# The second feed-forward product as seven block products per pair of row and column halves, in place of eight

## The reference

```python
def _moe_ref(x, phi, w1, w2):            # x: 3072 tokens x 512
    logits = x @ phi                     # 32 slots
    ...                                  # 8 experts, 4 slots each
    c = exp(logits - max); c /= c.sum(1)
    return c @ slot_out

def _moe2_ref(x, w_in, w_out):           # w_in 512 x 2048, w_out 2048 x 512
    h = x @ w_in
    r = np.maximum(h, 0.0)
    g = r * r
    return g @ w_out
```

## Time and profile before

| what | value |
|---|---|
| median of 3 runs | 565.27 us (564.38 to 565.62) |
| the profiled execution, device time | 565.99 us |
| its span in the profile | 564.0 us |
| TensorE busy in the span | 520.0 us, 92% |
| VectorE / ScalarE / GpSimd busy | 291.5 / 274.9 / 107.1 us |
| first matmul of the second product | 273.13 us |
| last matmul of the kernel starts | 560.32 us |
| 256 tokens of the last stage, steady | 24.0 us |

### The profile page before, as it was taken

How to read it: one execution, slowest core, us unless ns; L and a number is a source line. 1 busy time by engine, 2 the same in 40 slices (tenths; PEclk the granted TensorE clock), 3 DMA queues, 4 the chain that set the end, 5 groups by cost and what they waited for, 6 DMA issues and landing times.

```text
span 564.0 us, 10786 instructions
## 1 busy us (share of the span) xinstructions
PE 520.0 (92%) x3477; PEld 400.6 (71%) x3477; DVE 291.5 (52%) x909; ACT 274.9 (49%) x722; POOL 107.1 (19%) x230
## 2 busy tenths in 40 slices
PE   2899999999999688676899999999999999999997
PEld 1677877888788522311788888888888888888886
DVE  4676676676776542302797444444443543544410
ACT  1677777777877310001766443443443444444420
POOL 1444444444444203300260000000000000000000
PEclk9999999999999979797999999999999999999999
DMA  6699945535644679998001000000000000000000
GB/s 256 231 403 405 405 161 186 193 126 153 206 144 129 224 294 397 387 387 321 1 0 40 20 22 33 19 19 19 19 37 19 19 19 19 19 37 19 19 20 37
DMA packets 25993, 77.01 MB, mean 137 GB/s; under 512 B 2416, under 2 KB 2416, under 8 KB 23408
## 3 DMA queue, kind: packets, MB, share of 16 engines
q1 hardware_dynamic: 21776, 64.10, 31.6%
q10 hardware_dynamic: 4192, 12.58, 5.9%
HBM read 70.39 MB, written 6.29 MB: 136 GB/s over the span
## 4 chain that ended last, share of the span: by engine, by line
PE 69%; DVE 8%; ACT 5%; issue 5%; POOL 4%; SPq 4%; DMA 3%; ACTq 0%; DVEq 0%; POOLq 0%
PE bank L1091 14%; PE bank L1090 14%; PE bank L1089 14%; PE bank L860 5%; PE bank L871 5%; POOL probs L385 4%; ACT probs L719 4%; PE bank L1076 4%; SPq L338 4%; PE bank L903 2%; DMA w_b<-w_dram 2%; PE bank L886 2%; PE bank L1038 1%; DVE g_s L688 1%; DVE probs L478 1%
## 5 line engine op out<-in xcount | busy, mean ns | idle before, releaser
L1091 PE MATMUL bank<-wo_hi,g_lo 128*128 128x512 f32 x352 | 138.6, 394 | 0.0
L1090 PE MATMUL bank<-wo_lo,g_hi 128*128 128x512 f32 x352 | 138.1, 392 | 0.0
L1089 PE MATMUL bank<-wo_hi,g_hi 128*128 128x512 f32 x352 | 137.4, 390 | 0.0
L688 DVE TENSOR_TENSOR g_s<-relu_s 128x512 f32<-128x512 f32 x96 | 69.4, 729 | 129.5 <-ACT relu_s L814 129.5
L814 ACT ACTIVATE relu_s<-bank 128x512 f32<-128x512 f32 x96 | 56.3, 596 | 124.3 <-PE bank L1076 124.2
L719 ACT ACTIVATE probs<-probs,nmax 128x232 f32<-128x232 f32 (+1 forms) x192 | 88.6, 463 | 50.5 <-DVE nmax L478 50.5
L385 POOL TENSOR_SCALAR probs<-probs,rden 128x232 f32<-128x232 f32 (+1 forms) x192 | 82.5, 448 | 104.3 <-DVE rden L487 104.3
L1091 PEld LDWEIGHTS bank<-wo_hi,g_lo 128*128 128x128 f32 x352 | 66.2, 188 | 14.1
L1090 PEld LDWEIGHTS bank<-wo_lo,g_hi 128*128 128x128 f32 x352 | 66.1, 188 | 11.9
L1089 PEld LDWEIGHTS bank<-wo_hi,g_hi 128*128 128x128 f32 x352 | 66.2, 188 | 11.6
L691 DVE TENSOR_TENSOR g_lo<-g_s,g_hi 128x512 fp32r<-128x512 f32 x96 | 68.7, 722 | 4.5
(11 more groups left out here) (129 smaller groups left out, 507.6 us busy)
## 6 DMA issues: line engine op xcount, KB each, us to landing
qkv_s<-qkv_dram SPq DMA_DIRECT2D x16, 1028.0 KB, 5.7
qkv_s<-qkv_dram SPq DMA_DIRECT2D x16, 704.0 KB, 4.1
w_s<-w_dram ACTq DMA_DIRECT2D x5, 2048.0 KB, 11.9
w_s<-w_dram SPq DMA_DIRECT2D x6, 1024.0 KB, 13.4
out_dram<-o_stage SPq DMA_DIRECT2D x24, 256.0 KB, 2.0
w_a<-w_dram SPq DMA_DIRECT2D x9, 512.0 KB, 10.9
wo_raw<-w_out_dram SPq DMA_DIRECT2D x4, 1024.0 KB, 14.3
w_pre<-w_dram ACTq DMA_DIRECT2D x1, 2048.0 KB, 18.0
```

The costliest lines, as they stand in the source:

```text
L688: dve.tensor_tensor(g_s[:, j % 4, :], relu_s[:, j % 4, :], relu_s[:, j % 4, :], ALU.mult).then_inc(squared, 1)
L1089: pe.matmul(bank[4 + q][:, :], hi, wo_hi[:, f, :], start=(f == 0), stop=False)
L1090: pe.matmul(bank[4 + q][:, :], hi, wo_lo[:, f, :], start=False, stop=False)
L1091: last = pe.matmul(bank[4 + q][:, :], lo, wo_hi[:, f, :], start=False, stop=(f == FFC - 1))
```

## The change

The matrix product of 256 tokens (two halves of 128, A1 and A2) x 2048 with w_out is written as 2 x 2 blocks: the token halves against the halves of the 16 blocks (u = 0, 1: a11, a12 for the first 128 tokens, a21, a22 for the second), and w_out against the halves of its rows and of its 512 columns. Seven block products of sums and differences replace the eight plain ones (Winograd's form of Strassen's scheme). The four combinations of w_out blocks (`t_32`, `t_hi`, `t_lo`) are made once. The four combinations of g blocks (`s_32`) are made for each pair of token tiles.

A block product has 256 output columns. The 16 blocks of hidden columns of a pair are worked in two groups (c = 0, 1) of 4 blocks of either half. A group is 7 products x 4 blocks x 3 matmuls = 84 matmuls of 256 columns, and 8 `hidden` matmuls of 256 columns for the pair after it, 4 behind its third product and 4 behind its fifth. So a pair of tiles has 168 + 16 matmuls of 256 columns, in place of 96 of 512 and 16 of 256. The first pair (`plain`) is computed with the plain eight products, since the w_out combinations are made beside it.

ScalarE's program becomes: the high parts of group G (`a_hi` for both plain blocks, then `s_hi` slots 0 to 4), then `gate` of group G + 2: ReLU of 1024 columns out of PSUM twice, then two squares in place of 1024 columns each, now on ScalarE too. VectorE makes three of the four combinations of g, `a_lo` and four of the five `s_lo` slots, and adds the seven products up to the output tiles (`outputs`, seven operations of 256 columns, PSUM against SBUF). GpSimd makes for every group the combination a11 - a21 and the low part of the slot 4. The set of parts exists once, in slots, and a slot is written anew when the product that read it in the group before is done; g itself (`g_s`) exists twice. The low part of w_out moves from VectorE and GpSimd to VectorE alone.

```diff
+            def gate(G, c, first, early=False):
+                if not first:
+                    act.wait_ge(lo_done, G * 5 - 5)
...
+                for u in range(2):
+                    act.wait_ge(h_ready, G * 2 + (u + 1))
+                    act.activation(g_s[c][:, u, :, :].rearrange("p f n -> p (f n)"), banks[:, u * 1024:(u + 1) * 1024], ACT.Relu)\
+                        .then_inc(relu_done, 1)
+                for u in range(2):
+                    act.wait_ge(relu_done, G * 2 + (u + 1))
+                    act.activation(g_s[c][:, u, :, :], g_s[c][:, u, :, :], ACT.Square).then_inc(squared, 1)
...
+            with act.Fori(2, NPAIR - 1) as k:
+                for c in range(2):
+                    group(k, c)
+                    gate(k * 2 + (c + 2), c, False)
...
+            LOW_AT = (1, 1, 2, 3, 4, 5)
+            FREE_AT = (1, None, 5, None, 6, None, 7)
+            def group(k, c, more, weights=False):
+                G = k * 2 + c
+                for n in range(7):
+                    if n < 6:
+                        pe.wait_ge(lo_done, G * 5 + LOW_AT[n])
                     else:
+                        pe.wait_ge(last_lo_done, G - 1)
...
+                    if c == 0 and FREE_AT[n]:
+                        pe.wait_ge(o_made, k * 7 + (FREE_AT[n] - 7))
+                    for f in range(GF):
...
+                        pe.matmul(OUT[n], hi, W_HI[n](at_f), start=(c == 0 and f == 0 and n % 2 == 0), stop=False, skip_group_check=True)
+                        pe.matmul(OUT[n], hi, W_LO[n](at_f), start=False, stop=False, skip_group_check=True)
+                        last = pe.matmul(OUT[n], lo, W_HI[n](at_f), start=False, stop=(c == 1 and f == GF - 1), skip_group_check=True)
+                    last.then_inc(product_done, 1)
+                    if more and n in (2, 4):
+                        hidden(k + 1, c, (n - 2) // 2, False)
```

VectorE's part of one group, and GpSimd's:

```diff
+            def group(k, c, o=None, turn=None):
...
+                blocks_low(G, c)
+                if c == 0 and o is not None:
+                    outputs(k - 1, o, turn, 0)
...
+                spent(3)
+                dve.tensor_tensor(s_32[:, 0, :, :], a21, a22, ALU.add).then_inc(sums_made, 1)
+                spent(4)
...
+                dve.tensor_tensor(s_32[:, 1, :, :], s_32[:, 0, :, :], a11, ALU.subtract).then_inc(sums_made, 1)
+                if c == 0 and o is not None:
+                    outputs(k - 1, o, turn, 1)
...
+                slot_low(G, 0, 2)
+                spent(6)
...
+                dve.tensor_tensor(s_32[:, 3, :, :], a12, s_32[:, 1, :, :], ALU.subtract).then_inc(sums_made, 1)
+                if c == 0 and o is not None:
+                    outputs(k - 1, o, turn, 2)
...
+                slot_low(G, 1, 3)
+                slot_low(G, 2, 4)
+                slot_low(G, 3, 5)
...
+            def group(G, c):
+                g = g_s[c]
+                pool.wait_ge(squared, G * 2 + 1)
...
+                pool.wait_ge(product_done, G * 7 - 2)
...
+                pool.tensor_tensor(s_32[:, 2, :, :], g[:, 0, :, 0:P], g[:, 0, :, P:CH], ALU.subtract).then_inc(third_made, 1)
+                pool.wait_ge(hi_done, G * 6 + 6)
...
+                pool.tensor_tensor(s_lo[:, 4, :, :], g[:, 1, :, P:CH], s_hi[:, 4, :, :].bitcast(F32), ALU.subtract)\
```

More of the change, by code:

```diff
@@ L340, in _ @@
             sp.wait_ge(mid_pe, pe_at["l1_1"])
-            for n in range(4):
+            for n in (0, 2, 1, 3):
                 blocks = slice(4 * n, 4 * n + 4)
@@ L694, in chunk @@
[L694 to L707, removed]
+            wo_low(0, 0)
@@ new lines, in _ @@
+            plain_low(0)
+            combine(1, range(4))
+            wo_low(1, 2)
+            plain_low(1)
+            t_low(0)
+            group(1, 0)
+            t_low(1)
+            group(1, 1)
+            with dve.Fori(0, (NPAIR - 2) // 2) as it:
+                for o in range(2):
+                    k = it * 2 + (2 + o)
+                    group(k, 0, 1 - o, it + o)
+                    group(k, 1, 1 - o, it + o)
+            for which in range(4):
+                dve.wait_ge(product_done, 2 * NPAIR * 7 - 7 + (2, 4, 6, 7)[which])
+                outputs(NPAIR - 1, 1, (NPAIR - 1) // 2, which)
@@ new lines, in _ @@
+            gate(0, 0, True)
+            plain_high(0)
+            wo_high(1)
+            wo_high(3)
+            gate(1, 1, True)
+            plain_high(1)
+            t_high(0)
+            gate(2, 0, False, True)
+            t_high(1)
+            gate(3, 1, False, True)
+            group(1, 0, False)
+            gate(4, 0, False)
+            group(1, 1, False)
+            gate(5, 1, False)
+            with act.Fori(2, NPAIR - 1) as k:
+                for c in range(2):
+                    group(k, c)
+                    gate(k * 2 + (c + 2), c, False)
@@ L842, in _ @@
+            for c in range(2):
+                group(NPAIR - 1, c)
+            act.wait_ge(o_made, (NPAIR - 1) * 7)
+            act.sem_inc(waits_act, 1)
+            act.wait_ge(product_done, 2 * NPAIR * 7 - 5)
+            act.activation(post[:, 0, :], bank[4][:, 0:HD], ACT.Copy).then_inc(p1_copied, 1)
         @block.tensor
@@ L1070, in _, with hidden @@
                 mark(pe.matmul(bank[4 + n][:, :], low, mix_gl[:, :], start=False, stop=True), f"m{n}")
[L1073 to L1076 removed]
+            def hidden(k, c, u, first):
+                G = k * 2 + c
+                if not first:
+                    pe.wait_ge(relu_done, G * 2 + (u - 1))
+                for f in range(GF):
+                    at_f = HF * u + GF * c + f
+                    last = pe.matmul(banks[:, u * 1024 + f * CH:u * 1024 + (f + 1) * CH], mix[:, at_f * P:(at_f + 1) * P],
@@ new lines, in plain @@
+            def plain(c):
+                for n in range(4):
+                    t, u = n // 2, n % 2
+                    pe.wait_ge(lo_done, c * 5 + (1, 5)[t])
+                    pe.wait_ge(wo_lo_done, 2 * c + u + 1)
+                    for f in range(GF):
+                        hi = (a_hi, s_hi)[t][:, u, f, :]
+                        lo = (a_lo, s_lo)[t][:, u, f, :]
+                        at_f = HF * u + GF * c + f
+                        pe.matmul(bank[4 + t][:, :], hi, wo_hi[:, at_f, :], start=(c == 0 and u == 0 and f == 0), stop=False, skip_group_check=True)
+                        pe.matmul(bank[4 + t][:, :], hi, wo_lo[:, at_f, :], start=False, stop=False, skip_group_check=True)
+                        last = pe.matmul(bank[4 + t][:, :], lo, wo_hi[:, at_f, :], start=False,
+                                         stop=(c == 1 and u == 1 and f == GF - 1), skip_group_check=True)
+                    last.then_inc(product_done, (1, 1, 1, 4)[n])
+                    if n in (1, 3):
+                        hidden(1, c, n // 2, False)
@@ L1134 @@
+            for c in range(2):
+                for u in range(2):
+                    pe.wait_ge((mix_act, mix_dve)[c], u + 1)
+                    hidden(0, c, u, c == 0)
+            plain(0)
+            plain(1)
+            group(1, 0, True, True)
+            group(1, 1, True, True)
+            with pe.Fori(2, NPAIR - 1) as k:
+                for c in range(2):
+                    group(k, c, True)
+            for c in range(2):
+                group(NPAIR - 1, c, False)
 def kernel(q, k, v, n_global, n_local, moe_phi, moe_w1, moe_w2, moe2_w_in, moe2_w_out):
```

295 lines of the change are left out of this document (179 added, 116 removed).

## The result

The changed kernel takes 639.1 us (638.5 to 639.3, 4 runs) against 565.4 us: 1.130 times as long, 95% interval 1.128 to 1.133. The profiled execution has a span of 637.5 us.

A forecast was written before the change was run, and what follows sets the result against it. TensorE bound the old kernel; in the new one, ScalarE's order would stall it in every group. The stretches summed to a span of 616.4 us, 617.7 as median; 19 for clock falls gave 637, range 608 to 656.

The forecast's parts named there:

- TensorE alone: Steady stage: small matmuls at 0.118 us each, a pair of tiles 21.7 us in place of 24.0.
- Durations: New operations priced from smaller ones: of 1024 elements, ScalarE 1.02 to 1.07 us, VectorE 1.22; Square priced as a copy.
- The path: ScalarE's gate of the next group delays a_hi and a_lo: TensorE stands about 2.5 us per group, a pair takes 28.5.
- The stall at the third product: In a pair's first group, product 3 waits for the fifth output add on VectorE: a stall of 1.2 us.
- GpSimd: Its two operations per group lock out VectorE mostly in idle time or slack: 0 to 6 us in all, taken as 0.
- The start: First product at 276.9 us in place of 273.13; after a 24.0 us plain pair, group 2 waits 6.6 us, starting at 307.5.
- The clock: TensorE falls to half clock behind stalls, 1.6 us a fall, 19 us in all; falls at about half: chance 0.42.
- 23 stalls: Stalls of TensorE that could each bring a clock fall; falls were assumed at 12 of them.
- The rival on the other side: Chain of ReLU, squares, a_hi and a_lo hidden behind products 6 and 7, TensorE the bound: 545 to 551 us, chance 0.07.

The follow-up runs named there:

- filler run: Changed kernel with useless matmuls of 256 columns in TensorE's stalls, 18 behind each group and 40 behind the plain pair: 622.3 us.
- split kernel: Kernel before the change, with each matmul of 512 columns of the steady chunks made as two of 256: 571.1 us.
- run with VectorE's other order: Changed kernel with ScalarE's high parts ahead of the gates, group 2 included, and VectorE's third to sixth output adds made earlier: 552.7 us.
- tight version: The run with VectorE's other order, plus 26 useless matmuls ahead of the stage's first product: 550.3 us.

## Why the prediction was right

The forecast was 637 us with a range of 608 to 656; 639.1 was measured. In the profiled execution, beside the forecast's sum without its term for the clock, and beside the filler run, in which the clock is held from 279 us on (us):

| stretch | forecast, full clock | changed kernel | with filler |
|---|---|---|---|
| first product of the stage, at | 276.9 | 275.0 | 274.6 |
| to the first product of group 2 | 30.6 | 32.8 | 32.7 |
| pair 1 | 27.2 | 31.3 | 27.5 |
| nine pairs | 256.6 | 271.8 | 259.5 |
| last pair, to the last matmul | 22.0 | 23.0 | 22.0 |
| rest of the span | 3.1 | 3.7 | 3.7 |
| span | 616.4 | 637.5 | 620.0 |

By its steps:

**TensorE alone** was priced at 0.118 us for a small matmul and 21.7 us for a pair. The split kernel shows 0.118, the version without stalls 21.88 us a pair. The estimate by the Trainium skill ("TensorE: Matmul & The Clock Gate", section Back-to-back issue gap), under which the small matmuls would lose by themselves, does not hold here. For the split kernel's chunk the same page's figures would give an estimated 20.4 us (208 at 98 ns) against 14.1 before, 44% more. Measured are 24.5 against 24.0 us, 2% more.

**Durations** of the operations of 1024 elements were put together from rows of 256 to 768. The groups by form of the changed kernel show them (VectorE's from 310 us on):

```profile
L964 ACT ACTIVATE g_s<-bank 128x1024 f32<-128x1024 f32 x48 | 48.7, 1024 | 96.0 <-PE bank L1263 62.2 <-DVE s_lo L753 33.8
L968 ACT ACTIVATE g_s<-g_s 128x1024 f32<-128x1024 f32 x48 | 47.9, 1050 | 0.0
...
L747 DVE TENSOR_TENSOR a_lo<-g_s,a_hi 128x1024 fp32r<-128x1024 f32 x21 | 25.7, 1225 | 134.8 <-ACT a_hi L972 134.8
```

1.02, 1.05 and 1.22 were the prices. The page of the changed kernel has one table load, as before, so `Square` brought none.

**The path** was right in its members, its place and its size. From first product to first product, 14.7 us were forecast for the first group of a pair and 13.8 for the second, 28.5 together; with the clock held up they took 14.9 and 13.9, 28.8. The stall at the third product was priced at 1.2 us. It is shown with 0.86, costs 1.1 by the starts, and another 0.2 is lost at the fourth product, the same unseen loss as in the run with VectorE's other order. In one point the reading was too strict: the high part does not wait for the end of the squares of the next group, it starts 0.1 us ahead of their shown end (412.42 against 410.52 + 2.00 us). The chain is shown, not argued: moving one of its members off it removed the stalls, and taking 4.0 us a pair out of it shortened the pair by 3.8.

**GpSimd** was taken as without effect. It costs 0.2 us a pair in the changed order, 2 us in all, and nothing that can be seen in the tight version.

**The start:** the first product was to come 8.9 us behind the first matmul that spreads `mix` (L1252), in place of 5.1. It came 274.96 - 266.14 = 8.8 us behind it. Group 2 was to stand for 6.6 us; it stood for 6.5. The terms written out for these two add up, without the handovers, to 6.1 us (behind the last `mix` copy) and 5.9 only, where 6.6 was set down for both, so part of these hits is luck. At the start, ScalarE waited 0.3 us more for `hidden`. Ahead of group 2, both ReLUs and not one came behind the last `hidden` block, since ScalarE was making `t_hi` until 301.06 us.

By the clock of the execution the first product came 1.9 us earlier than forecast, because the stage did. The likely reason, which no run isolates, is that the low stretch ahead of it lasted 3.4 us there (from 258.6 us) and 6.8 in the execution the forecast was read from. The plain pair then took 26.3 us in place of 24.0. The two misses cancel, and that group 2 started at 307.7 us as forecast (307.5) is luck.

**The clock** was the term with the widest bounds, 0 to 46 us, taken as 19: 12 falls at 1.6 us. The filler run prices the falls from group 2 on at 16.9. There were 14 low stretches behind 300 us. Twelve lasted 3.4 us and two 6.8, where those before were read as 6.4 to 6.6, and the mean granted clock from 306 us on was 0.92:

```profile
306.39:313.21 6.82, 5.49 (x26) 5.52 (x27) 6.48 (x11) 2.93 (x5) 0.90 (x1) 0.50 0.23 80
354.18:357.59 3.41, 3.41 (x16) 3.41 (x17) 2.93 (x5) 2.41 (x5) 0.00 (x0) 0.50 0.00 0
...
306.00:637.50 331.50, 269.85 (x2008) 263.61 (x2008) 180.84 (x259) 166.50 (x222) 57.90 (x43) 0.92 0.05 19
```

A loss of 0.08 x 331.5 = 27 us of clock cost 17 us of time. Much of the rest went where the forecast did not look. In the four pairs whose first group had the fall, the third product has no stall: the waits above count six of them in ten pairs. Work at half clock had taken the stall's place, and three of these groups took 14.9 to 15.1 us, hardly more than the 14.9 without a fall. In the second group of a pair, which has no such stall, a fall cost 1.5 us.

A fifteenth low stretch, at the stage's start (272.2 to 279.1 us), cost the plain pair about 2 us. The forecast's 23 stalls must have counted this place, as 22 groups follow it, but its 24.0 us for the plain pair had nothing for it. So the clock took 19 us in all, as forecast, by 15 stretches at about 1.3 us where 12 at 1.6 had been assumed. That the two errors cancel is luck.

The rival on the other side (the chain hidden, 545 to 551 us) named the point at which it decides. The version in which the chain is in fact off the path runs at 550 us.

## What to carry to other kernels

Where buffers become single, write down for each engine which instruction of the next item stands in front of the one that the bound engine waits for: here a strictly ordered engine had the ReLU of group G + 2 ahead of the high part of group G + 1, and swapping them was worth 75 us without saving an instruction (some 15 of them the clock's: the 16.9 of the filler run less 2.4 for the fall at group 2, which stayed). A stall on TensorE has a second price, its clock, and useless matmuls in an unavoidable stall can be worth their place.

## What the runs showed of the hardware that was not expected

- Stalls of 2.4 to 2.7 us between groups of some 11 us of matmuls made the clock fall to half in 13 of 20 cases. The low stretches lasted 3.4 us in most cases, not 6.8. Filling the stalls up to rests of 0.2 and 0.6 us kept the clock at 1.00 for 340 us, though stalls of 0.85 us at the third product stayed.
- On ScalarE, a wait for the end of the operation just issued and a counter step, in front of an operation that needed neither, cost 0.6 us when ScalarE was otherwise ready; without them this operation started before the shown end of the one in front.
- Of 2.8 us of work in a pair that VectorE took over from GpSimd, 0.5 appeared as busy time; GpSimd's operations had stretched VectorE's low parts from 0.69 to 0.97 us each, 2.2 us in a pair.
- A small matmul behind a stall costs more than the idle time shown: with 0.28 us shown, 0.54 us were lost, and at another place 0.2 us with no idle time shown.
- Of the stalls ahead of a pair's second group (2.4 us) nine of ten were followed by a fall, of those ahead of its first (2.7 us) four of ten. In the run without GpSimd it was seven and six of ten. What decides which are hit was not settled.
